# A linear-attention + gated-MLP kernel: layer 1 of the first two blocks in 256-token sets, a new dealing of dense steps, VectorE's scaling of R in one instruction

## The reference, cut to what matters

```python
# r, k, v, w: (batch 4, heads 8, seq 768, head_dim 48), u: (8, 48)
for t in range(S):
    cur = einsum('bhd,bhe->bhde', u[None] * k_t, v_t)
    y[:, :, t] = einsum('bhd,bhde->bhe', r_t, state + cur)
    state = w_t[..., None] * state + einsum('bhd,bhe->bhde', k_t, v_t)
x = y.transpose(0, 2, 1, 3).reshape(3072, 384)
gate = 1 / (1 + exp(-(x @ w_gate)))          # w_gate, w_val: (384, 1536)
x = (gate * (x @ w_val)) @ w_out             # layer 1, w_out: (1536, 384)
h = x @ w2_in                                # (384, 2048)
out = where(h > 0, h, exp(min(h, 0)) - 1) @ w2_out   # layer 2, (2048, 384)
```

## Time and profile before

| | |
|---|---|
| median of three runs | 1200.02 us |
| the profiled execution | 1203.46 us, its span 1201.7 us |
| TensorE matmul busy | 1155.2 us, 96% of the span |
| TensorE weight loads busy | 1006.1 us, 84% |
| VectorE busy | 667.4 us, 56% |
| ScalarE busy | 472.0 us, 39% |
| GpSimd busy | 294.0 us, 24% |
| mean granted TensorE clock | 0.986 of 2.4 GHz |

### The profile page before, as it was taken

One profiled execution on the slowest core, in us unless ns is written; L12 is line 12 of the kernel. 1 busy time (PEld: TensorE's weight loads), 2 busy tenths in 40 slices (PEclk: granted clock), 3 DMA queues, 4 the chain that ended last, 5 costly groups with the idle time before them and its releaser, 6 DMA issues.

```text
span 1201.7 us, 16511 instructions
## 1 busy us (share of the span) xinstructions
PE 1155.2 (96%) x6336; PEld 1006.1 (84%) x6336; DVE 667.4 (56%) x1044; ACT 472.0 (39%) x889; POOL 294.0 (24%) x290
## 2 busy tenths in 40 slices
PE   5778998999999999999999999999999999999999
...
DMA packets 153454, 52.39 MB, mean 44 GB/s; under 512 B 126624, under 2 KB 148768, under 8 KB 153376
## 3 DMA queue, kind: packets, MB, share of 16 engines
...
## 4 chain that ended last, share of the span: by engine, by line
PE 80%; DVE 13%; issue 4%; ACT 2%; DMA 0%; POOL 0%; DVEq 0%; POOLq 0%; ACTq 0%
PE ps L606 21%; PE ps L639 17%; PE ps L631 16%; PE ps L615 10%; DVE RKW L828 7%; PE ps L544 6%; PE ps L560 3%; PE ps L534 3%; PE ps L565 2%; PE ps L573 2%; DVE A L853 1%; DVE work L907 1%; DVE WL L893 1%; DVE WS L917 1%; DVE hl L897 1%
## 5 line engine op out<-in xcount | busy, mean ns | idle before, releaser
L606 PE MATMUL ps<-xh,WS 128*128 128x512 f32 x864 | 251.2, 408 | 1.6 <-DVE xl L888 1.6
L669 ACT ACTIVATE hh<-work 128x512 fp32r<-128x512 f32 x168 | 106.5, 634 | 287.0 <-DVE work L907 202.5
L544 PEld LDWEIGHTS ps<-RKW 128*128 128x128 f32 x1152 | 157.3, 203 | 57.9 <-DVE RKW L828 49.8
L544 PE MATMUL ps<-RKW 128*128 128x128 f32 x1152 | 168.1, 293 | 32.9 <-DVE RKW L828 32.5
L639 PE MATMUL ps<-WS,hh 128*128 128x384 f32 x768 | 198.0, 339 | 0.5 <-DVE hl L897 0.5
L828 DVE TENSOR_TENSOR RKW<-RKW,WL 64x256 f32<-64x256 f32 x288 | 183.3, 636 | 16.1 <-PE ps L544 13.6
L897 DVE TENSOR_TENSOR hl<-work,hh 128x512 fp32r<-128x512 f32 x168 | 132.9, 791 | 88.3 <-ACT hh L669 87.7
L606 PEld LDWEIGHTS ps<-xh,WS 128*128 128x128 f32 x864 | 155.1, 190 | 30.7 <-issue 1.8
L631 PE MATMUL ps<-xh,WS 128*128 128x512 f32 x576 | 164.2, 397 | 0.0
L615 PE MATMUL ps<-hh,WS 128*128 128x512 f32 x432 | 161.6, 411 | 0.4 <-DVE hl L897 0.3
L934 DVE SCALAR_TENSOR_TENSOR work<-work,ps 128x512 f32<-128x512 f32 x96 | 66.0, 688 | 169.6 <-ACT work L757 169.6
...
## 6 DMA issues: line engine op xcount, KB each, us to landing
nat<-in_w_dram SPq DMA_DIRECT2D x24, 192.0 KB, 3.7
nat<-in_k_dram SPq DMA_DIRECT2D x24, 192.0 KB, 4.9
nat<-in_r_dram SPq DMA_DIRECT2D x24, 192.0 KB, 5.3
V<-in_v_dram SPq DMA_DIRECT2D x24, 192.0 KB, 4.5
...
RKW<-in_moe_w_in_dram SPq DMA_DIRECT2D x16, 192.0 KB, 2.4
```

Of the source, the lines that this page charges most:

```text
L544: last = mm(bank[b][:, p * P:(p + 1) * P].rearrange("p (e i l) -> p e i l", e=2, l=L), K[:, g, :], Rb[:, :, :, 1, :], start=True, stop=True)
L606: last = mm(ps[:, VAL if val else GATE, :], gate_w(a, val, j, c), xp[b][:, c, :], start=(i == 0 and c == 0), stop=(i == 2 and c == KC - 1))
L669: return nc.scalar.activation(o, i, ACT.Copy)
```

## The change

**Sets.** Layer 1 no longer runs by blocks but by sets: blocks 0 and 1 make four sets of one half each (256 columns), blocks 2 to 5 one set each (512 columns). Eight sets, m = 0 to 7. A 256-column set has the same 324 matmuls, with the same weights, half as wide. `transpose_x(m)` takes the place of XT, and the x2 scratch is stored half by half.

**Order.** Only q0 runs alone. Set 0 runs beside q1, set 1 beside q2 and 8 parts of q3, set 2 beside the rest of q3 and 16 parts of q4, set 3 beside the rest of q4 and q5. From set 4 (block 2) on all is dealt as before. Beside the 256-column sets a part gets dense thirds by `SHARE`: 5 for L1 to L3, 4 for L4, 2.5 for L5 and L6, 2 for the transposes, 1 or 0.5 for KT, Y and S.

**Weights of layer 1.** Six splits are in q0 (behind L5, L6, KT), the other 30 behind the groups of set 0. The first eight pieces have raw buffers of their own (six in `work`, two in `Yt`), then the ring of four as before.

**R.** `R` is stored by head of a pair first, and VectorE scales both heads in one instruction over 128 partitions and 512 elements (half of them zeros), in place of two over 64 partitions and 256 elements. The last level keeps two.

**Start.** The loads of r, k and w wait for nothing; only the padding of `nat` is cleared. GpSimd clears `R` and `A`.

```diff
+    HALVED = 2
+    TH = U * P
+    SETS = [(n, (hf,)) for n in range(HALVED) for hf in range(HALF)] + [(n, (0, 1)) for n in range(HALVED, NB)]
+    MORE = {1: 8, 2: 16}
+    def spread(dense, parts, room, share=None):
+        share = [share[part[2]] if share and part[0] == "a" else 1 for part in parts]
+        steps = []
+        for i, third in enumerate(dense):
+            steps.append(third)
+            steps += [parts[s] for s in range(len(parts)) if int(sum(share[:s]) * room / sum(share)) == i]
+        return steps
+    SHARE = {"Tw": 2, "Tk": 2, "Tr": 2, "L1": 5, "L2": 5, "L3": 5, "L4": 4, "L5": 2.5, "L6": 2.5, "KT": 1, "Y": 0.5, "S": 0.5}
+    for m in range(NS):
+        beside = STREAM[done:STREAM.index(("x", m + 1)) + 1 + MORE.get(m, 0)] if m + 1 < NS else []
+        if beside and beside[-1][0] == "x" and SETS[m + 1][1] == (0, 1):
+            PROGRAM += spread(THIRDS[m], beside[:-1], len(THIRDS[m]) - 3, SHARE if len(SETS[m][1]) == 1 else None) + [beside[-1]] + LATE[m]
+        else:
+            PROGRAM += spread(THIRDS[m], beside, len(THIRDS[m]) - 1, SHARE) + LATE[m]
+    EARLY = [("a", 0, name, b) for name in ("L5", "L6", "KT") for b in range(U)]
+        NR1, ONCE = 4, 4
...
                     for c in range(KC):
-                        last = mm(ps[:, VAL if val else GATE, :], gate_w(a, val, j, c), xp[b][:, c, :],
+                        last = mm(ps[:, VAL if val else GATE, t], gate_w(a, val, j, c), xp[b][:, c, t],
                                   start=(i == 0 and c == 0), stop=(i == 2 and c == KC - 1))
...
-                for e in range(2):
-                    rows = slice(e * HP, (e + 1) * HP)
-                    Rb = blocks(R[rows, pairs, e, :], L)[:, :, :, 1, :]
-                    out_R = blocks(RP[rows, pairs, :], L)[:, :, :, 1, :] if li == NL - 1 else Rb
-                    last = tt(out_R, Rb, Wb[rows, :, :, 0].to_broadcast([HP, PR, P // (2 * L), L]), ALU.mult)
+                Rb = R[:, :, pairs].rearrange("q e g (i two l) -> q e (g i) two l", two=2, l=L)[:, :, :, 1, :]
+                if li < NL - 1:
+                    last = tt(Rb, Rb, Wb.unsqueeze(1).unsqueeze(3).to_broadcast([P, 2, n, L]), ALU.mult)
...
-                nc.vector.memset(nat[:, x], 0.0).then_inc(d_zero, 1)
+                pads = nat[:, x].rearrange("p g (e d) -> p (g e) d", e=2)[:, :, D:HP]
+                nc.vector.memset(pads, 0.0).then_inc(d_zero, 1)
```

More of the change, by code:

```diff
@@ L91, in build, with splits @@
+    assert done == len(STREAM)
+    N1 = 3 * F1
+    EARLY = [("a", 0, name, b) for name in ("L5", "L6", "KT") for b in range(U)]
+    AHEAD = len(EARLY)
+    def splits(step):
+        return step in EARLY or (step[:2] == ("d", 0) and step[-1] == 2)
+    SPLIT1 = {step: x for x, step in enumerate([step for step in PROGRAM if splits(step)][:N1])}
+    SPLIT2 = {("d", NS - 1, "v", j + 1, 2): j for j in range(F1 - 2)}
+    assert len(SPLIT1) == N1
     DOWNS = F2 - 1 + B
@@ L332, in _ @@
-            load_shift(v, 1, 0)
+            load_v(0)
+            load_shift(v, 0)
+            load_w1(0, NR1 + ONCE)
+            load_half(1)
+            load_v(1)
+            load_w1(NR1 + ONCE, 2 * NR1 + ONCE)
+            load_shift(k, 1)
+            load_shift(v, 1)
             def split_until(step):
-                return AHEAD + sum(x[0] != "a" and x[-1] == 2 for x in MIXED[:MIXED.index(step)])
-            at = [NR1 + AHEAD] + [NR1 + split_until(("a", hf, name, 1)) for hf, name in ((0, "L4"), (0, "Y"), (1, "L4"))] + [N1]
+                return sum(PROGRAM.index(x) < PROGRAM.index(step) for x in SPLIT1)
@@ L374, in _ @@
                 load_w2(j)
-            store_x2(NB - 1)
-            sp.wait_ge(x2_stored, 16 * (NB + 1))
-            for i in range(0, NB - 1):
-                load_x2(i + 1)
-                store_out(i)
+            store_x2(NS - 1)
+            for n in range(NB - 1):
+                load_x2(n + 1)
+                store_out(n)
             for b in range(B):
@@ L986, in _ @@
+                if step == ("d", NS - 1, "v", F1 - 1, 2):
+                    split_x(0)
+            for n in range(NB):
                 for step in STEPS2:
-                    layer2(i, *step, True)
-            for step in STEPS2:
-                layer2(NB - 1, *step, False)
+                    layer2(n, *step)
+                    if n == 0 and step in LATE2:
+                        split_w2(F1 - 2 + LATE2.index(step))
 _INS = ["r", "k", "v", "w", "u", "moe_w_gate", "moe_w_val", "moe_w_out", "moe2_w_in", "moe2_w_out"]
```

569 lines of the change are left out of this document (254 added, 315 removed).

## The result

The changed kernel takes 1192.31 us (median of four runs, 1191.60 to 1193.12), the one before 1199.07 on the same chip (four runs, 1197.89 to 1201.31): a ratio of 0.9942, 95% interval 0.9924 to 0.9959. The interval excludes 1, so the change is faster, by 6.8 us where 24 were forecast.

The account below looks back on a forecast made before the run. TensorE was taken to bound the full stages, with waits for VectorE and a lower clock at the start; saving 86.3 - 49.7 (S0) - 12.3 (W) = 24.3 us, 1200.0 - 24.3 = 1175.7, stated as 1176, range 1164 to 1192.

Parts of the forecast that it names:

- W: All waits of TensorE from the first dense matmul of set 0 to the start of block 2: 12.3 us.
- Pace of narrow matmuls: Layer 1 of blocks 0 and 1: a 256-column matmul takes 0.117 us, half of the 0.2345 for 512 columns.
- The slower rival: Narrow matmuls of blocks 0 and 1 don't halve: the change loses from 0.136 us each, 1251 us at 0.175; chance 0.07.
- TensorE's need: TensorE's work from the first dense matmul of set 0 to the start of block 2: 265.3 us.
- S0: Time of the first dense matmul, after q0 and x0: 49.7 us, range 45 to 53.
- One scaling for two: VectorE's merged scaling of R costs 0.91 us where a pair cost 1.27: 4.4 us per half, 2.6 off S0.
- W, set 0: In set 0's levels VectorE needs 33.0 us against TensorE's 25.9: 7.3 us of waits, 14 if the clock drops.
- Late weight piece: In set 0, behind L4 of q1, ScalarE waits for a weight piece behind q2's loads: 2 us (0 to 5).
- Handovers: Passing x to the sets, x1 and x4 with only 2.1 us of matmuls to hide them: 3 us (0 to 6).
- Sets 1 to 3 without a wait: In set 1 VectorE needs about 18.0 us against TensorE's 20.2, so no wait; sets 2 and 3 alike.
- VectorE sets the pace of set 0: Rival: VectorE needs 59 of TensorE's 61 us throughout set 0, which takes 74; 1182 to 1185 us; chance 0.2.
- The start shrinks more: Rival: scalings hardly wait and splits use idle time, S0 46, W 6: saving 34 us, 1166; chance 0.12.

Follow-up runs that it names:

- e3: The kernel before with only R stored by head first and scaled by one instruction, nothing else of the change: 1179.24 us, ratio 0.9824.
- e2: The changed kernel with the scaling of R done again as pairs of instructions: 1215.83 us, ratio 1.0136.
- e7: e1 with VectorE clearing the low parts of the weights from the seventh piece on instead of subtracting: 1175.37 us, ratio 0.9794.
- e17: e1 with GpSimd's diagonal terms formed on only 4 of 48 columns of each head: 1165.95 us, ratio 0.9712.
- e1: The changed kernel with the last two weight pieces of layer 1 loaded ahead of q2's loads: 1188.17 us, ratio 0.9894.
- e8: e1 with all parts beside the narrow sets dealt evenly (SHARE 1 for every stage): 1186.08 us, ratio 0.9881.

## Why the prediction was wrong

The failed step is W, the waits of the sets: 12.3 forecast, 22.9 + 7.3 + 4.0 + 1.1 = 35.3 measured. The sum stands otherwise: 46.5 + 263.1 + 35.3 = 344.9, and block 2 begins at 345.0.

- **Pace of narrow matmuls.** Right: 0.118 (forecast 0.117). The slower rival, 0.136 and up, is refuted. The Trainium skill's 0.109 for it ("TensorE: Matmul & The Clock Gate", Back-to-back issue gap and LDWEIGHTS), from a formula that the page gives for an isolated matmul, is 8% under the measurement, as at 512 columns; the measurement decides. TensorE's need was 263.1, forecast 265.3.
- **S0.** 46.5, forecast 49.7, better than the sum. But its terms were off: R was priced at 2.6. e3 shows up to 8.7 for q0 and q1 together, nearer the whole 4.4 per half than 60% of it, and with it a fuller clock. e2 has S0 at 58.4 with pairs, in its slowest execution.
- **One scaling for two.** Price right (forecast 0.91, measured 0.863 and 0.911 for its two forms), worth far too small: 21 us alone. Left out were its effect in the first mixed stage (9.2 us, of which I booked nothing on its own) and in each full stage (1.8, "nothing off TensorE is worth anything"). The sign of what the rest of the change does was therefore wrong too: the R part gives nearly what I forecast for the whole, and the sets take 13.5 back.
- **W, set 0.** I took 7.3, the price of 6.4 us of excess in the first mixed stage, and named 14 "if the clock drops". It did: 10.9 of waits and up to 10.0 of clock. The step that failed is the transfer of that price. There TensorE came back from each wait at full clock in most of the stage (0.97); here the waits for a piece, for a split and for a scaling fall into one stretch (105 to 110), and 13.7 us at half clock follow. The mechanism was right in part: VectorE is behind with its splits, and e7 shows it with the late piece: both away, 15.3 us come back. But I had it act through the levels ("waits of L566 for L821 of about 7 us"), and that wait is 3.7. The other 7.2 us are waits of the dense groups: 3.2 for the rest of h, for which the sum has no term, 2.7 for a split behind the late piece, 1.3 for the rest of x and a product. What holds VectorE longest, GpSimd's long instructions, stood in the sum only as a mean of 0.21 us per instruction; e17 shows 12.9 us of set 0 for them, with the clock.
- **Late weight piece.** Named at 2 us (0 to 5); it waits 3.6 and stands in the chain, and its cure alone gives 1.8 of set 0 and 4.1 in the medians (e1). Right in place; wrong as a term that adds.
- **Handovers.** 3 us together were forecast; the waits for the rest of x at the heads of sets 0 and 1 are 1.0 and 0.9, in sets 2 and 3 there is none.
- **Sets 1 to 3 without a wait.** Wrong for 1 and 2: 7.3 and 4.0. "Some 18.0 against 20.2" left 2.2 us of slack in means, but the means hide instructions held for 1.7 to 2 us by GpSimd. e17 takes 2.7 and 2.5 us off the two; e8's even dealing takes 3.1 off set 1. What remains of their loss, beside waits for the rest of h (L629, 2.6 us in set 1), wasn't split further.
- **The rival "VectorE sets the pace of set 0"** (W 18 to 20, 1182 to 1185) was nearest in kind, but had no clock in it and nothing for sets 1 and 2. "The start shrinks more" was right on S0 and wrong on W.
- **Late in the program.** Block 5 and layer 2 unchanged, as forecast.

Against the forecast of 24.3 us: W -23.0, S0 +3.2, TensorE's need +2.2, three full stages +5.4: 12.1, and the spans differ by 11.8. The medians differ by 6.8, as the execution before that I read from was above its median by 4.4 (3.4 by the runs shown then, which I had taken off) and the one profiled after is 0.7 below.

Open: what (e), the short groups, costs by itself. No run had GpSimd's terms and the splits away at once. In e17, with the terms short and the clock full in set 0, the matmuls of the "o" groups still wait 3.1 us there and 1.8 in set 1 for the rest of h.
